# Fetching the first expert tile's rows directly, and the order of the routing operations, in a fused attention and two-MoE kernel

## The reference, cut to what matters

```python
def _attn_ref(q, k, v, s):            # batch 2, heads 8, 576 positions, head size 64
    scores = scale * q @ k.T;  bias = -(cum[:, None] - cum[None, :]);  causal mask; softmax; @ v

def _moe_ref(x, w_gate, w1, w2):      # x: 1152 tokens x 512; 8 experts, hidden size 1024
    logits = x @ w_gate
    expert_idx = np.argmax(logits, axis=1)
    gate_w = probs[np.arange(N), expert_idx]          # probs: softmax of the logits
    for e in range(E):
        mask = expert_idx == e
        out[mask] = gate_w[mask, None] * (np.maximum(x[mask] @ w1[e], 0.0) @ w2[e])

def _moe2_ref(x, domain_probs, w1, w2):               # 4 experts, all tokens through each
    p = domain_probs / (domain_probs.sum(-1, keepdims=True) + 1e-09)
    for e in range(E):
        out += p[:, e:e + 1] * (np.maximum(x @ w1[e], 0.0) @ w2[e])
```

## Time and profile before

| what | us |
|---|---|
| median of 3 runs | 772.53 (771.75 to 774.69) |
| the profiled execution, its own time | 771.7 |
| its span, first to last instruction | 769.9 |
| attention, until TensorE's last matmul of it | 142.1 |
| from there to the first matmul of the first expert tile | 28.7 |
| the eight expert tiles | 190.2 |
| the second mixture and the end | 408.9 |

### The profile page before, as it was taken

One profiled execution on the slowest core, in us unless ns is written; L12 is line 12 of the kernel. 1 busy time (PEld: TensorE's weight loads), 2 busy tenths in 40 slices (PEclk: granted clock), 3 DMA queues, 4 the chain that ended last, 5 costly groups with the idle time before them and its releaser, 6 DMA issues.

```text
span 769.9 us, 14486 instructions
## 1 busy us (share of the span) xinstructions
PE 733.8 (95%) x5044; PEld 664.1 (86%) x5045; DVE 307.5 (40%) x804; ACT 263.9 (34%) x632; POOL 154.3 (20%) x174
## 2 busy tenths in 40 slices
PE   6989999789999999998999999999999999999996
PEld 5777777579999999998999989999999999999995
DVE  4787777505545455544431324312144121212211
ACT  2777776105545445553321113211132111111110
POOL 4666566131221221221110001100001000001001
PEclk9899999899999999999999999999999999999998
DMA  7735513146656677654420003300030000001001
GB/s 185 218 93 156 162 29 108 49 147 191 192 183 183 192 210 215 192 191 145 138 82 1 1 1 107 113 0 0 0 82 27 0 0 0 0 0 41 14 27 41
DMA packets 56054, 71.46 MB, mean 93 GB/s; under 512 B 33968, under 2 KB 33968, under 8 KB 55504
## 3 DMA queue, kind: packets, MB, share of 16 engines
q1 hardware_dynamic: 54384, 65.01, 28.8%
q0 software_dynamic: 1456, 4.76, 1.7%
q10 hardware_dynamic: 176, 1.22, 0.4%
HBM read 65.78 MB, written 5.19 MB: 92 GB/s over the span
## 4 chain that ended last, share of the span: by engine, by line
PE 88%; issue 3%; SPq 2%; DVE 2%; DMA 1%; POOL 1%; DVEq 1%; ACT 1%; ACTq 0%
PE bank L1134 26%; PE wide L1145 26%; PE wide L1097 11%; PE bank L1085 9%; PE bank L1021 4%; PE bank L1003 3%; PE wide L955 3%; PE bank L986 1%; POOL x_slots L472 1%; PE wide L960 1%; PE bank L1066 1%; PE wide L929 1%; DMA stages<-in_moe_w 1%; SPq L288 1%; DVEq L848 1%
## 5 line engine op out<-in xcount | busy, mean ns | idle before, releaser
L1134 PE MATMUL bank<-x2Th,w_hi 128*128 128x384 f32 (+1 forms) x384 | 129.2, 337 | 2.0 <-DVE x2Tl L840 2.0
L1134 PE MATMUL bank<-x2Tl,w_hi 128*128 128x384 f32 (+1 forms) x384 | 129.4, 337 | 0.0
L1134 PE MATMUL bank<-x2Th,w_lo 128*128 128x384 f32 (+1 forms) x384 | 128.9, 336 | 0.0
L481 POOL TENSOR_TENSOR w_lo<-stages,w_hi 128x1024 fp32r<-128x1024 f32 x22 | 52.5, 2388 | 380.4 <-ACT w_hi L606 380.4
L1085 PE MATMUL bank<-xT,w_hi 128*128 128x192 f32 x512 | 96.5, 280 | 6.0 <-DVE h1T L832 3.7
L1097 PE MATMUL wide<-h1T,w_hi 128*128 128x192 f32 x512 | 94.2, 275 | 0.0
L606 ACT ACTIVATE w_hi<-stages 128x1024 fp32r<-128x1024 f32 x88 | 92.7, 1053 | 0.0
L824 DVE TENSOR_TENSOR w_lo<-stages,w_hi 128x1024 fp32r<-128x1024 f32 x66 | 80.8, 1224 | 23.7 <-ACT w_hi L606 23.4
L1085 PEld LDWEIGHTS bank<-xT,w_hi 128*128 128x128 f32 x512 | 83.2, 195 | 7.8 <-DVE h1T L832 4.8
L638 ACT ACTIVATE h_0h<-bank 128x384 fp32r<-128x384 f32 x48 | 23.6, 492 | 188.3 <-PE bank L1134 188.3
L873 DVE SCALAR_TENSOR_TENSOR h_0l<-bank,h_0h 128x384 fp32r<-128x384 f32 x48 | 26.8, 558 | 141.1 <-ACT h_0h L638 141.1
(11 more groups left out here) (164 smaller groups left out, 1248.9 us busy)
## 6 DMA issues: line engine op xcount, KB each, us to landing
stages<-in_moe_w SPq DMA_DIRECT2D x96, 512.0 KB, 4.1
cum_bc<-cum_dram SPq DMA_DIRECT2D x3, 1152.0 KB, 9.3
x_rows<-x_slots SPq DMA_DIRECT2D x9, 256.0 KB, 2.9
q_nat<-in_q SPq DMA_DIRECT2D x16, 128.0 KB, 2.6
k_nat<-in_k SPq DMA_DIRECT2D x16, 128.0 KB, 3.7
v_nat<-in_v SPq DMA_DIRECT2D x16, 128.0 KB, 2.6
cum_bc<-cum_dram ACTq DMA_DIRECT2D x1, 1152.0 KB, 8.0
x_rows<-x_slots SPq DMA_DIRECT2D x9, 128.0 KB, 3.0
```

The source lines that it names most:

```text
L481: g.tensor_tensor(w_lo[par][:, c], stage[3][:, :], w_hi[par][:, c].bitcast(F32), ALU.subtract).then_inc(lo_done[3], 1)
L1134: last = te.matmul(bank[ft % 2][:, 0:CHUNK], w1_of((w_hi, w_lo)[st][par], kk, ft * P, P), x_mv, start=(n == 0), stop=(n == 11))
```

## The change

1. The finished rows of `x_nat` are also stored in token order to a new DRAM tensor `x_dram`, by seven DMAs on SyncE (`store_x`): two ahead of the second expert's first weight pieces, five behind them, each of these after its row block of the last units.
2. As soon as the ranks are there, VectorE makes for each of the ten blocks a 0/1 matrix `in_first` of 192 columns: column n is 1 for the token whose rank in expert 0 is n. Twenty small matmuls of these with the token numbers (`token_parts`, in two parts that bf16 holds exactly) give the token number of each slot of the first tile. VectorE turns them into integers (`first_id`), and two indirect DMAs on GpSimd fetch the 2 x 96 rows from `x_dram` into `x_first`. They stand ahead of the ten scatters. TensorE's first `turn_x` reads `x_first`, and its second one the rows that SyncE loads from `x_slots`.
3. The logits of the first batch, and six heads of the second, are summed during the attention's last steps (`partial_logits`); the sum at the start of the routing has 120 elements in place of 640. `valid` replaces two clearing operations; the shifted logits, the counts per expert and the counts' matmul move behind the point where the ranks' matmuls can start.
4. `keep_clock_wide` runs 16 matmuls, not 80. All tiles are turned in two halves of 96 rows, not 128 and 64, and a tile's rows come by one DMA, not two.
5. Four more `iota` operations on GpSimd and a few memsets on VectorE at the start; `x_nat` lies elsewhere in SBUF.

The core of the diff:

```diff
+            def store_x(b_, i0, i1):
+
+                rows = slice(b_ * S + START[i0], b_ * S + START[i1 - 1] + ROWS[i1 - 1])
+                sp.dma_start(x_dram[rows, :].rearrange("(i p) d -> p i d", p=ROWS[i0]),
+                             x_nat[0:ROWS[i0], b_ * NT + i0:b_ * NT + i1, 0:DM]).then_inc(m["x_stored"], 16)
+
+            sp.wait_ge(m["norm_done"], 2 * PAIR_UNITS)
+            store_x(0, 0, 1)
+            store_x(0, 1, NT)
             W1S, W2S = range(4), range(4, PIECES)
             stream(1, 1, W1S)
+            for i in range(NT):
+                sp.wait_ge(m["norm_done"], 3 * PAIR_UNITS + NT + (i + 1))
+                store_x(1, i, i + 1)
...
-                for g, n in enumerate(TURN_ROWS):
-                    sp.dma_start(x_rows[0:n, g, :], x_slots[bass.ds(row + g * P, n), 0:DM]).then_inc(m["x_rows_loaded"], 16)
-
-            load_rows(0)
+                sp.dma_start(x_rows[:, :, :], x_slots[bass.ds(row, TOK), 0:DM].rearrange("(g p) d -> p g d", p=ROWS_T)).then_inc(m["x_rows_loaded"], 16)
+
             sp.dma_start(pay[:, :, :], x_slots[0:N, DM:XROW].rearrange("(t p) c -> p t c", p=P)).then_inc(m["p2_loaded"], 16)
...
+            pool.wait_ge(m["x_stored"], 16 * (2 + NT))
+            pool.wait_ge(m["first_id_ready"], 1)
+            for g_ in range(TURNS):
+                pool.indirect_dma_start(x_first[:, g_, :], None, x_dram[:, :],
+                                        bass.IndirectOffsetOnAxis(first_id[0:ROWS_T, g_:g_ + 1], 0)).then_inc(m["first_loaded"], 16)
...
+                if n == PAIR_UNITS:
+                    partial_logits()
+
+            def by_expert(r0, h0, h1):
+                return head_logits[:, r0:r0 + NT, h0 * E1:h1 * E1].rearrange("p r (h e) -> p r e h", h=h1 - h0)
+
+            def partial_logits():
+
+                dve.wait_ge(m["norm_done"], 3 * PAIR_UNITS + NT)
+                ve.tensor_reduce(r_["lg"][:, 0:NT, :], by_expert(0, 0, H), AX.X, ALU.add).then_inc(m["partial_logits"], 1)
+                ve.tensor_reduce(head_logits[:, NT:RT, H * E1:LOGITS], by_expert(NT, 0, H - 2), AX.X,
+                                 ALU.add).then_inc(m["partial_logits"], 1)
 
             iterations(step, 3, dve)
...
-            then(ve.tensor_reduce(r_["lg"][:, :, :], head_logits[:, :, :].rearrange("p r (h e) -> p r e h", h=H), AX.X, ALU.add))
+            dve.wait_ge(m["partial_logits"], 2)
+            then(ve.tensor_reduce(r_["lg"][:, NT:RT, :], by_expert(NT, H - 2, H + 1), AX.X, ALU.add))
...
-            for b_ in range(B):
-                then(ve.memset(r_["one"][64:P, b_ * NT, :], 0.0))
-            then(ve.tensor_copy(onehot[:, :, :], r_["one"][:, :, :]))
-            then(ve.tensor_reduce(e_["cnt"][:, :], r_["one"][:, :, :].rearrange("p r e -> p e r"), AX.X, ALU.add))
-            ve.tensor_copy(oh_sum[:, :], e_["cnt"][:, :]).then_inc(m["onehot_ready"], 1)
+            dve.wait_ge(m["sums_cleared"], 4 + B)
+            ve.tensor_tensor(onehot[:, :, :], r_["one"][:, :, :], valid[:, :, :], ALU.mult).then_inc(m["onehot_ready"], 1)
+            ve.tensor_tensor(r_["sh"][:, :, :], lg, over_e(mx), ALU.subtract).then_inc(m["shift_ready"], 1)
+            dve.wait_ge(m["onehot_ready"], 1)
+            then(ve.tensor_reduce(e_["cnt"][:, :], onehot[:, :, :].rearrange("p r e -> p e r"), AX.X, ALU.add))
+            ve.tensor_copy(oh_sum[:, :], e_["cnt"][:, :]).then_inc(m["counted"], 1)
+            dve.wait_ge(m["rank_ready"], 1)
+            rank = bank[2][:, 0:RT * E1].rearrange("p (r e) -> p r e", r=RT)
+            then(ve.scalar_tensor_tensor(out=first_slot[:, :], in0=rank[:, :, 0], scalar=1.0, in1=onehot[:, :, 0],
+                                         op0=ALU.add, op1=ALU.mult))
+            for r in range(RT):
+                ve.tensor_scalar(in_first[:, r, :], slot_row[:, :], first_slot[:, r:r + 1], None,
+                                 ALU.is_equal).then_inc(m["first_ready"], 1)
 
             dve.wait_ge(m["ex_done"], 1)
             then(ve.tensor_reduce(c_["sum"][:, :], r_["ex"][:, :, :], AX.X, ALU.add))
             then(ve.tensor_scalar(c_["eps"][:, :], c_["sum"][:, :], TINY, None, ALU.add))
             then(ve.reciprocal(x_nat[:, :, GATE], c_["eps"][:, :]))
-            dve.wait_ge(m["rank_ready"], 1)
-            rank = bank[2][:, 0:RT * E1].rearrange("p (r e) -> p r e", r=RT)
-            then(ve.tensor_copy(e_["all"][:, :], bank[2][:, 256:256 + E1]))
+            dve.wait_ge(m["token_psum"], 1)
+            ve.tensor_reduce(first_token[0:ROWS_T, :], half[3][0:ROWS_T, 0:2 * TURNS].rearrange("p (g v) -> p g v", v=2), AX.X,
+                             ALU.add).then_inc(m["first_step"], 1)
+            dve.wait_ge(m["first_step"], 1)
+            ve.tensor_copy(first_id[0:ROWS_T, :], first_token[0:ROWS_T, :]).then_inc(m["first_id_ready"], 1)
+            dve.wait_ge(m["count_ready"], 1)
+            then(ve.tensor_copy(e_["all"][:, :], half[2][:, 0:E1]))
...
-            te.matmul(bank[2][:, 256:256 + E1], ones[:, :], oh_sum[:, :], start=False, stop=True,
-                      skip_group_check=True).then_inc(m["rank_ready"], 1)
-
+                last = te.matmul(bank[2][:, d * E1:RT * E1], ones[:, :], oh[:, 0:(RT - d) * E1], start=False,
+                                 stop=(d == RT - 1), skip_group_check=True)
+            last.then_inc(m["rank_ready"], 1)
+            pe.wait_ge(m["counted"], 1)
+            te.matmul(half[2][:, 0:E1], ones[:, :], oh_sum[:, :], start=True, stop=True,
+                      skip_group_check=True).then_inc(m["count_ready"], 1)
+            for r in range(RT):
+                pe.wait_ge(m["first_ready"], r + 1)
+                for g_ in range(TURNS):
+                    last = te.matmul(half[3][0:ROWS_T, 2 * g_:2 * g_ + 2], in_first[:, r, g_ * ROWS_T:(g_ + 1) * ROWS_T], token_parts[:, r, :],
+                                     start=(r == 0 and g_ == 0), stop=(r == RT - 1), skip_group_check=True)
+            last.then_inc(m["token_psum"], 1)
 
             def keep_clock_wide(times):
                 with pe.Fori(0, times // 8) as _:
@@ -1056,17 +1127,18 @@
                         te.matmul(bank[3][:, :], w_hi[0][:, 0:P], w_hi[0][:, 0:512], start=True, stop=True, skip_group_check=True)
 
             pe.wait_ge(lo_done[0], 2)
-            keep_clock_wide(80)
-
-            def turn_x(t):
-
-                pe.wait_ge(m["x_rows_loaded"], t * 32 + 32)
-                for g, n in enumerate(TURN_ROWS):
+            keep_clock_wide(16)
+
+            def turn_x(rows):
+
+                for g_ in range(TURNS):
                     for c in range(KD):
-                        last = te.transpose(turn_bank(g)[:, c, :], x_rows[0:n, g, c * P:(c + 1) * P], ident[0:n, 0:n])
+                        last = te.transpose(turn_bank(g_)[:, c, :], rows[:, g_, c * P:(c + 1) * P], ident[0:ROWS_T, 0:ROWS_T])
                     last.then_inc(m["xT_psum"], 1)
 
-            turn_x(0)
+            pe.wait_ge(m["route_ready"], 3)
+            pe.wait_ge(m["first_loaded"], 16 * TURNS)
+            turn_x(x_first)
...
-                turn_x(t + 1)
+                pe.wait_ge(m["x_rows_loaded"], t * 16 + 16)
+                turn_x(x_rows)
```

More of the change, by code:

```diff
@@ L51 @@
 MAXT = N // TOK
+ROWS_T = TOK // 2
+LOGITS = (H + 1) * E1
 LAG = 3
@@ L127, in moe_chain_kernel @@
             inv = [sb(f"inv{i}", [P, 2], F32, a) for i in range(2)]
-            x_nat = sb("x_nat", [P, RT, XROW], F32, a)
             zeros = sb("zeros", [P, XROW], F32, a)
             turn_gate = sb("turn_gate", [P, KD, OUTW], F32, a)
-            head_logits = sb("head_logits", [P, RT, H * E1], F32, a)
+            head_logits = sb("head_logits", [P, RT, LOGITS], F32, a)
+            valid = sb("valid", [P, RT, E1], F32, a)
+            slot_row = sb("slot_row", [P, TOK], F32, a)
+            first_slot = sb("first_slot", [P, RT], F32, a)
+            in_first = sb("in_first", [P, RT, TOK], BF16, a)
+            token_parts = sb("token_parts", [P, RT, 2], BF16, a)
+            first_token = sb("first_token", [P, 2], F32, a)
+            first_id = sb("first_id", [P, 2], I32, a)
+            x_first = sb("x_first", [ROWS_T, 2, DM], F32, a)
             r_ = {n: sb("r_" + n, [P, RT, E1], F32, a) for n in ("lg", "eq", "val", "one", "sh", "ex", "pos")}
@@ L163, in moe_chain_kernel @@
             slots_zeroed wg_loaded r_step ex_done onehot_ready rank_ready route_ready scattered payload_in
+            x_stored partial_logits shift_ready counted count_ready first_ready token_psum first_step first_id_ready first_loaded
             hi_done x_rows_loaded xT_psum xT_hi xT_lo h1_psum h1_hi h1_lo x2_psum x2_hi x2_lo
@@ L205, in down_pair @@
             return wide[pr][:, :].rearrange("p (a k) -> p a k", a=2)[:, :, 0:TOK]
-        TURN_ROWS = (P, TOK - P)
+        TURNS = 2
         def tile_start(off, j):
@@ L313, in _ @@
             load_v(0, 1, wait=False)
-            sp.wait_ge(m["consts"], 16)
+            sp.wait_ge(m["consts"], 20)
             for hh in range(2):
```

(20 more changed lines are left out.)

14 lines of the change are left out of this document (7 added, 7 removed).

## The result

The changed kernel takes 796.96 us (median of four runs, 795.18 to 798.71) against 772.42 us for the kernel before on the same chip: a ratio of 1.031, 95% interval 1.029 to 1.033. It is 24.5 us slower, where 763.1 and "faster" were forecast. The profiled execution took 798.3 us, with a span of 796.5.

The account below looks back on a forecast made before the run. Bound: the stretch from 142.1 to 170.8 us between attention and expert tiles, where TensorE does little useful. 771.7 - 14.7 (earlier tile) + 4.2 (stall) + 1.5 (clock) = 762.7, plus half of 0.8: 763.1 us; range 760 to 766, overall 757.5 to 768.

Parts of the forecast that it names:

- Elsewhere: Outside the reworked stretch: the four iota, early stores and later tiles' loads and transposes cost nothing; bound +0.8 us.
- The slower rival: Scatters beside the first tile: GpSimd's descriptor work advances only while VectorE rests, stall 20 us, total 779 us; chance 5%.
- Routing and fetch: From the logits' sum to the first tile's rows: integers ready at 148.4 us, rows landed at 153.4, 14.5 us earlier.
- the sums moved forward: Logit sums in the attention's last steps: hidden while VectorE waits for TensorE; at most 1.3 us if uncovered.
- The fetch: GpSimd's indirect loads of the first tile's rows: start after 0.93 us, second issue 1.36 later, landing 2.74 after that.
- First tile: Start of the first expert tile: 2.80 us from transposes to first matmul, less 0.2, so 14.7 us earlier, at 156.1.
- The late piece: Second expert's weight piece 4, queued on SyncE behind the scatters: issued at 170.2, landed at 174.1; ScalarE waits 7.8 us.
- The stall before up 7: TensorE in the first tile, waiting on late weights: up 7 at 176.8 instead of 172.7, 4.2 us; bounds 1.5 to 7.
- the prediction's own clock term: TensorE's slower clock after the stall in the first tile: 1.5 us taken, bounds 0 to 1.9.
- rival 2: Scatters beside the first tile: GpSimd waits three times behind L824, scatters end up to 3.7 us later, 766.8 us; chance 15%.
- the rule that the prediction weighed: GpSimd and VectorE share an SBUF port pair; one instruction holds it while the other is blocked, lengthening scatters beside the tile.
- The sum: Whole kernel: 771.7 - 14.7 + 4.2 + 1.5 = 762.7, plus half of 0.8, gives 763.1 us; chance 50%.

Follow-up runs that it names:

- experiment 3: The changed kernel with the 44 clock-keeping matmuls at the attention's start written as a loop of two times 22: 763.81 us, ratio 0.9877.
- experiment 4: The changed kernel with the second expert's weight pieces 4 to 6 sent by SyncE before its wait for the scatters: 794.69 us, ratio 1.0281.
- +200: The kernel before with 100 small matmuls (200 instructions) added ahead of TensorE's expert loop: 779.15 us.
- +256: The kernel before with 128 small matmuls (256 instructions) ahead of TensorE's expert loop and 64 repeated matmuls in place of 80: 771.93 us, ratio 0.9988.
- +20: The kernel before with 10 small matmuls (20 instructions) added ahead of TensorE's expert loop: 801.85 us.
- +40: The kernel before with 20 small matmuls (40 instructions) added ahead of TensorE's expert loop: 805.56 us, ratio 1.0435.
- +128: The kernel before with 64 small matmuls (128 instructions) added ahead of TensorE's expert loop: 823.72 us.

## Why the prediction was wrong

**The step that failed** is "Elsewhere". It priced the `iota`, the stores and the loads that move, and took it that TensorE's later tiles run as before. It counted the twenty small matmuls as time (hidden beside `in_first`, which held) and not as places in TensorE's program. They pushed the loop over an edge, at 33.2 us by experiment 3. None of the rivals had this. The slower rival, GpSimd advancing only while VectorE rests, did not happen: the scatter of 159.70 took 0.98 us although an L888 ran beside it from 160.06, and the last one was issued 1.2 us later than forecast, not 16.

**Routing and fetch: right in kind, 1.0 us short.** The ranks' matmuls start at 144.57 (144.7 forecast), the sums moved forward are hidden, `first_id` ends at 148.60 (148.4). In that, `in_first` took 2.38 us and not 1.8: a step of 0.23 each (0.32 in duration) where 0.18 was taken, so the slope of the earlier trace rows was the wrong guide for so short an operation; 0.3 of the excess came back, since it began at 145.22 and not at 145.5. The fetch is where 0.8 was lost: first issue 0.91 us after its number (0.93 taken), second issue at 150.92, rows there at 154.4, a landing of 3.4 us, the upper bound, where 2.74 was taken. First tile at 157.13 (156.1).

**The late piece: right.** SyncE's DMA issues in order of time (answers to the earlier trace rows):

```profile
168.26 0.38 SPq L388 DMA_DIRECT2D pay<-x_slots  x1
170.95 0.37 SPq L386 DMA_DIRECT2D x_rows<-x_slots  x1
171.70 16.93 SPq L197 DMA_DIRECT2D stages<-in_moe_w  x8
```

Piece 4 goes out 14.6 us after the tile's start (14.1 forecast), 3.5 us after the scatters are in (4.0). ScalarE, in order of time, waited 8.5 us for it (7.8 forecast, against the earlier trace rows):

```profile
175.94 1.06 ACT L643 ACTIVATE w_hi<-stages 128x1024 fp32r<-128x1024 f32 x1 [8.54 <-DMA stages<-in_moe_w]
```

The stall before up 7 was 4.84 (4.2 forecast), and up 7 took 2.88 at half clock for 1.34. The twelve matmuls behind it took 2.02 for 1.34, so the clock cost 2.2 us there, over the 1.5 taken and over its bound of 1.9. Experiment 4 shows the cause of the stall, since it goes with the order of the issues. Between the first and the second tile are 31.5 us, where 29 were forecast (24.9 and the stall; the prediction's own clock term is not in the 29).

**GpSimd beside VectorE: rival 2 in part.** The scatters were forecast to be in at 166.2 and are at 168.2; 0.2 of it is the later start; the rest is the last three, 1.1 in their issues and 0.7 in the last one's own landing (3.47 for 2.74). GpSimd and VectorE in order of time, 160 to 166 us of the changed kernel:

```profile
159.70 0.98 POOL L508 DMA_INDIRECT x_slots<-x_nat,slot_of  x1 [0.30 <-issue]
160.98 1.14 POOL L508 DMA_INDIRECT x_slots<-x_nat,slot_of  x1 [0.30 <-issue]
162.43 2.00 POOL L508 DMA_INDIRECT x_slots<-x_nat,slot_of  x1 [0.30 <-issue]
164.74 1.70 POOL L508 DMA_INDIRECT x_slots<-x_nat,slot_of  x1 [0.30 <-issue]
```

```profile
160.06 1.22 DVE L888 TENSOR_TENSOR w_lo<-stages,w_hi 128x1024 fp32r<-128x1024 f32 x1 [0.59 <-ACT w_hi L643]
...
162.36 1.23 DVE L888 TENSOR_TENSOR w_lo<-stages,w_hi 128x1024 fp32r<-128x1024 f32 x1 [0.58 <-ACT w_hi L643]
...
164.36 1.23 DVE L888 TENSOR_TENSOR w_lo<-stages,w_hi 128x1024 fp32r<-128x1024 f32 x1 [0.51 <-ACT w_hi L643]
```

A scatter that begins while an L888 runs waits for its end and then takes 0.84 us: 161.28 - 160.98 + 0.84 = 1.14; 163.59 - 162.43 + 0.84 = 2.00; 165.59 - 164.74 + 0.84 = 1.69. One that began ahead of it (159.70) is not slowed. In experiment 4 it is the same three times (1.22, 2.00 and 1.70 us). In experiment 3 two scatters start 0.2 to 0.3 us ahead of an L888 and run beside it, at 0.97 each (the second begins 0.1 us before the end of the L888 ahead, too little to tell); the third begins within one and takes 163.80 - 163.56 + 0.84 = 1.08:

```profile
161.02 0.97 POOL L508 DMA_INDIRECT x_slots<-x_nat,slot_of  x1 [0.30 <-issue]
162.29 0.97 POOL L508 DMA_INDIRECT x_slots<-x_nat,slot_of  x1 [0.30 <-issue]
163.56 1.08 POOL L508 DMA_INDIRECT x_slots<-x_nat,slot_of  x1 [0.30 <-issue]
```

```profile
161.19 1.21 DVE L888 TENSOR_TENSOR w_lo<-stages,w_hi 128x1024 fp32r<-128x1024 f32 x1
...
162.59 1.21 DVE L888 TENSOR_TENSOR w_lo<-stages,w_hi 128x1024 fp32r<-128x1024 f32 x1
```

So the rule that the prediction weighed (the Trainium skill, SBUF — State Buffer, Who interferes with whom: whoever issues first has the shared pair for the whole instruction, and the other is blocked) is borne out in one direction, for an operation with two SBUF inputs. In the other it is not: the L888 of 160.06 begins while a scatter runs and takes its usual 1.22 us. What the prediction had against the rule, the nine scatters of the earlier trace rows, says nothing on it, as their neighbours read PSUM.

**The sum.** Without the gaps (experiment 3) the kernel takes 763.81 where the working gave 763.1. The closeness is partly luck. In that kernel's profile the first tile starts 14.0 us earlier than before (14.7 forecast) and lasts 32.05 us for 24.89, which is 7.2 more (5.7 forecast: the stall was 5.3, and the clock after it cost 2.7). Those two misses, 2.2 us, are made up by the seven later tiles: from the start of the second to the second mixture it is 163.3 us where it was 165.6, 2.3 less, for which "Elsewhere" had nothing. One part of it is seen in the rows: a later tile's eight transposes take 0.66 us for 0.82.

## What to carry to other kernels

Before adding instructions ahead of a long loop, count how many pieces of code the loop touches and where it starts in one (only TensorE's loop was tested here), and compare q8 of the page before and after. The stall with "issue" as its releaser at each return of the loop was cured here by moving the loop (rolling up something ahead of it), and not by the data flow (experiment 4). And when work leaves the critical path, list all who wait for it: here the weights behind the wait made the first tile last 31.5 us instead of 24.9, which took back 6.6 of the 13.6 us by which it came earlier.

## What the hardware showed beyond that

- A loop of 6.6 pieces of 16 KB on TensorE is kept or lost as a whole: from starts 0, +200 and +256 it returns without fetching again (with one wait of 1.15 us, at the first return of +200), and from +20, +40 and +128 with gaps of 7.6 to 8.1 us (7.8 to 8.2 in the changed kernel). In the changed kernel nine transfers are fetched for each return, more than the loop has pieces, which looks like each piece being put out before its turn comes; that part was only argued. The Trainium skill speaks, in section Instruction fetch mechanics of the page Runtime: NRT & Kernel Launch, of a fetch whenever a taken branch leaves a window of two pages; the kernel before, which jumps back over 6.6 pieces with no transfer on q8 from 219 to 365 us, disagrees, and the runs decide. The same section gives TensorE room for 2,048 instructions, which is eight such pieces; the runs are nearer to that, but lose the loop where by the count above it touches eight. Which pieces count (415 instructions twice are never run), and why +128 waits a second time in every round, stays open.
- An indirect DMA's issue on GpSimd is held at its start by a VectorE operation that reads two SBUF tensors, by up to 1.16 us, and not once it has begun; the VectorE operation is not held by it.
- The last scatter lands 7.1 us after its issue began when 1.5 MB of weight pieces were sent ahead of the wait (experiment 4); it is 3.5 without them and 2.74 in the earlier trace rows.
